# Linear attention in two chained feed-forward stages: the queries' maxima taken by VectorE transposes, and the keys' chain put ahead of them

## What is computed

```python
def phi(x):                                   # per head: 576 x 64 -> 576 x 256
    proj = x @ w_phi                          # 64 x 128
    proj = proj - max(abs(proj), axis=-1)
    return concat([exp(proj), exp(-proj)])
q_p, k_p = phi(q), phi(k)
kv  = einsum('bhsf,bhsd->bhfd', k_p, v)
z   = sum(k_p, axis=tokens)
att = (q_p @ kv) / (q_p @ z + 1e-06)          # heads side by side: 576 x 512
# first feed-forward stage (x_prev is x shifted by one token)
xk = mu_k * x + (1 - mu_k) * x_prev;  xr = mu_r * x + (1 - mu_r) * x_prev
y  = sigmoid(xr @ w_r) * (relu(xk @ w_k) ** 2 @ w_v)
# second stage: 512 -> 1024, a convolution over 3 tokens as a gate, 1024 -> 512
h = relu(y @ w_in);  out = (h * sigmoid(conv3(h))) @ w_out
```

## Time and profile before

| | us |
|---|---|
| median of 3 runs | 1418.75 (1409.08 to 1427.29) |
| the profiled execution | 1417.62 |
| its span | 1415.8 |
| TensorE busy (PE) | 1360.0 (96%) |
| VectorE busy (DVE) | 672.6 (48%) |
| ScalarE busy (ACT) | 626.6 (44%) |
| mean granted TensorE clock | 0.984 |
| first tile matmul of batch 0 starts at | 94.37 |
| second phase starts at about | 990 |

### The profile page before, as it was taken

One profiled execution on the slowest core, in us unless ns is written; L12 is line 12 of the kernel. 1 busy time (PEld: TensorE's weight loads), 2 busy tenths in 40 slices (PEclk: granted clock), 3 DMA queues, 4 the chain that ended last, 5 costly groups with the idle time before them and its releaser, 6 DMA issues. The chain is left out here.

```text
span 1415.8 us, 26326 instructions
## 1 busy us (share of the span) xinstructions
PE 1360.0 (96%) x10368; PEld 1211.6 (86%) x10368; DVE 672.6 (48%) x1047; ACT 626.6 (44%) x1111; POOL 13.5 (1%) x18
## 2 busy tenths in 40 slices
PE   5879999999999999999999999998899999999998
PEld 4668899889888889888988888998788988998997
DVE  5444244334433624442544362451757556655753
ACT  3536345454352534545445353443444443433532
POOL 0000000000000000000000000000300000000000
PEclk9879999999999999999999999999999999999999
DMA  5411202202212120220221212030310210110101
GB/s 165 124 45 40 58 27 77 63 20 69 61 45 70 40 58 26 62 78 19 70 54 53 69 41 58 25 116 22 93 64 1 71 64 30 41 63 30 41 30 38
DMA packets 94579, 78.60 MB, mean 56 GB/s; under 512 B 64656, under 2 KB 72976, under 8 KB 93456
## 3 DMA queue, kind: packets, MB, share of 16 engines
q1 hardware_dynamic: 94480, 77.10, 18.2%
HBM read 57.75 MB, written 19.02 MB: 54 GB/s over the span
## 5 line engine op out<-in xcount | busy, mean ns | idle before, releaser
L472 PE MATMUL psm<-xk_hi,wk_hi 128*128 128x288 f32 x512 | 158.6, 310 | 15.1 <-issue 6.9
L969 PE MATMUL psh<-y_hi,win_hi 128*128 128x288 f32 x512 | 153.9, 301 | 13.4 <-ACT h L1054 9.0
L818 DVE TENSOR_TENSOR k_lo<-square,k_hi 128x288 fp32r<-128x288 f32 x128 | 58.7, 458 | 221.3 <-ACT square L683 221.3
L472 PE MATMUL psm<-k_hi,wv_hi 128*128 128x288 f32 x512 | 154.4, 302 | 0.0
L472 PE MATMUL psm<-xk_lo,wk_hi 128*128 128x288 f32 x512 | 153.7, 300 | 0.0
L472 PE MATMUL psm<-xk_hi,wk_lo 128*128 128x288 f32 x512 | 153.2, 299 | 0.0
L970 PE MATMUL psh<-y_lo,win_hi 128*128 128x288 f32 x512 | 152.2, 297 | 0.0
L971 PE MATMUL psh<-y_hi,win_lo 128*128 128x288 f32 x512 | 151.6, 296 | 0.0
L472 PE MATMUL psm<-k_lo,wv_hi 128*128 128x288 f32 x512 | 151.1, 295 | 0.0
L472 PE MATMUL psm<-k_hi,wv_lo 128*128 128x288 f32 x512 | 150.8, 295 | 0.0
L1112 DVE SCALAR_TENSOR_TENSOR conv<-h,taps,conv 128x576 f32<-128x576 f32 x64 | 55.2, 863 | 141.3 <-ACT conv L1056 141.3
(11 more groups left out here) (116 smaller groups left out, 2810.9 us busy)
## 6 DMA issues: line engine op xcount, KB each, us to landing
v_nat<-in_v SPq DMA_DIRECT2D x32, 320.0 KB, 3.6
qk<-in_q SPq DMA_DIRECT2D x32, 288.0 KB, 2.9
qk<-in_k SPq DMA_DIRECT2D x32, 288.0 KB, 3.2
den<-den_scr SPq DMA_DIRECT2D x64, 144.0 KB, 3.0
y_scr<-y SPq DMA_DIRECT2D x64, 144.0 KB, 1.8
y<-y_scr SPq DMA_DIRECT2D x8, 1152.0 KB, 5.5
out<-rows SPq DMA_DIRECT2D x32, 256.0 KB, 2.0
den_parts<-den_rows SPq DMA_DIRECT2D x128, 2.2 KB, 1.9
```

The source lines that it names most:

```text
L472: return nc.tensor.matmul(o, lhsT, rhs, start=first, stop=last)
L818: nc.vector.tensor_tensor(k2_lo[:, i, :], square[:, i % 2, :], k2_hi[:, i, :].bitcast(F32), ALU.subtract).then_inc(k2_lo_ready, 1)
L969: nc.tensor.matmul(o, wh, xh, start=first, stop=False, skip_group_check=True)
```

## The change

- `QP`, `M`'s five transposes, `P0` and `P1` go. A new TensorE step `E` (`features_and_keys`) makes the queries' features once, with features on partitions (512 + 64 columns for each head), together with the ten key matmuls, which are woven between them. Three waits on `shared_bank` inside it keep writes to one bank apart.
- The keys' chain comes first on VectorE (`shift_keys`): maximum and subtraction of the two tail blocks (256 elements), then of the eight other blocks (1024 elements).
- The queries' maxima: `QT` (`part_maxima`) on VectorE: two 32x32 block transposes of 576 elements a partition out of PSUM, a reduction over 1152 elements, a copy of 64; then `M`: one TensorE transpose of 128x128; then `spread_maxima` on VectorE: a reduction over 128 elements, a cast, a subtraction, and a product over 576 elements that makes `max_blocks`. ScalarE's copy of the maxima goes.
- `KV` stands right behind `M`, ahead of `PICK`, whose input VectorE makes in `spread_maxima`; then `PICK` (`subtract_maxima`): four matmuls over the full height of the array, 512 + 64 + 64 + 512 columns, which add the negative maxima to the features. Then four exponentials, one for each head and sign (2 x 2 of 576 elements as before).
- `DEN` and `NUM` work on chunks of 64 + 512 and 512 + 64 columns in place of 288 + 288. The denominator is copied only when `NUM` is through.
- The list of steps becomes E, QT, EK, M, KV, PICK, DEN, NUM, with tiles behind E, EK, PICK (3200 ns each: two tiles) and NUM (1600: one tile), and 4000 in place of 6000 ns of tiles ahead of the first. Nothing of batch 1 is done in the front any more.

```diff
-FILL_NS = {"QP": 2200, "M": 1600, "P0": 3500, "P1": 2600}
-FIRST_FILL, LAST_FILL, RC_AFTER, DV_AFTER = 6000, 1600, 3500, 9000
+FILL_NS = {"E": 3200, "EK": 3200, "PICK": 3200, "NUM": 1600}
+FIRST_FILL, RC_AFTER, DV_AFTER = 4000, 3800, 9500
...
-        steps += [(s, p) for s in ("KP", "M", "EK", "P0", "KV", "P1", "DEN", "NUM")]
+    return [(s, p) for p in range(PAIRS) for s in ("E", "QT", "EK", "M", "KV", "PICK", "DEN", "NUM")]
...
+        def features_and_keys(p, a):
...
+            key_tile(0, TT - 1).then_inc(shared_bank, 1)
+            feature_chunk(1, 1, True)
+            feature_chunk(0, 0, True)
+            await_(pe, shared_bank, 3 * PAIRS, a, 3 * p + 1)
+            key_tile(1, TT - 1).then_inc(shared_bank, 1)
+            key_tile(0, 0)
+            key_tile(1, 0)
+            await_(pe, shared_bank, 3 * PAIRS, a, 3 * p + 2)
+            feature_chunk(0, 1, True).then_inc(shared_bank, 1)
+            key_tile(1, 1)
+            key_tile(0, 1)
+            await_(pe, shared_bank, 3 * PAIRS, a, 3 * p + 3)
+            feature_chunk(1, 0, False).then_inc(raw_features, 1)
+            for t in range(2, TT - 1):
+                for h in range(2):
+                    last = key_tile(h, t)
+            last.then_inc(k_projected, 1)
...
+        def part_maxima(p, a):
+            for h in range(2):
+                nc.vector.transpose(q_turn[:, h, :], q_cols(h, p, a)).then_inc(q_turned, 1)
+            await_(dve, q_turned, 2 * PAIRS, a, 2 * p + 2)
+            await_(dve, max_turned, PAIRS, a, p)
+            nc.vector.tensor_reduce(q_part[:].rearrange("p (h c) -> p h c", h=4)[:, 0:2, 0:TOK],
+                                    q_turn[:].rearrange("p h (j f) -> p h j f", f=32), AX.X, ALU.max,
+                                    apply_absolute_value=True).then_inc(q_part_once, 1)
+            await_(dve, q_part_once, PAIRS, a, p + 1)
+            nc.vector.tensor_copy(q_part[:, P // 2:P], q_part[:, 0:P // 2]).then_inc(q_part_ready, 1)
+
+        def spread_maxima(p, a):
+            await_(dve, max_turned, PAIRS, a, p + 1)
+            nc.vector.tensor_reduce(q_max[:], turned_max(p, a).rearrange("q (i t) -> q t i", i=4), AX.X, ALU.max).then_inc(q_max_ready, 1)
...
+            await_(dve, features, PAIRS, a, p)
+            nc.vector.tensor_tensor(max_blocks[:], own_block[:].unsqueeze(2).to_broadcast([P, TOK, 32]),
+                                    q_max_split[:].bitcast(F32).unsqueeze(1).to_broadcast([P, TOK, 32]), ALU.mult).then_inc(blocks_ready, 1)
...
+            for h in range(2):
+                for chunk in CHUNKS[h]:
+                    cols = slice(*chunk)
+                    last = mm(q_cols(h, p, a)[:, cols], pick[:, h, :], max_blocks[:].rearrange("q j t -> q (j t)")[:, cols], False, True)
...
         def copy_den(p, a):
-            await_(act, den_summed, PAIRS, a, p + 1)
+            await_(act, attended, PAIRS, a, p + 1)
...
-                if m is None and kind in ("QP", "KP", "P1") and pieces < len(PIECES):
+                if m is None and kind in ("M", "KV", "NUM") and pieces < len(PIECES):
```

More of the change, by code:

```diff
@@ L48, in attention_steps @@
 def attention_steps():
-    steps = [("QP", 0)]
-    for p in range(PAIRS):
-        steps += [(s, p) for s in ("KP", "M", "EK", "P0", "KV", "P1", "DEN", "NUM")]
-        steps += [("QP", p + 1)] if p + 1 < PAIRS else []
-    return steps
+    return [(s, p) for p in range(PAIRS) for s in ("E", "QT", "EK", "M", "KV", "PICK", "DEN", "NUM")]
 def first_attention_steps():
-    steps = [("QP", 0), ("KP", 0)]
+    steps = [("E", 0)]
     for p in range(PAIRS):
         last = p == PAIRS - 1
-        def ahead(s):
-            return [(s, 0, "next") if last else (s, p + 1)]
         def before(s):
             return [(s, p - 1)] if p else []
-        steps += [("M", p)] + before("RC") + [("P0", p), ("EK", p)] + ahead("QP")
-        steps += [("KV", p), ("P1", p)] + before("DV") + ahead("KP") + [("DEN", p), ("NUM", p)]
+        steps += [("EK", p), ("QT", p)] + before("RC") + [("M", p), ("KV", p), ("PICK", p)] + before("DV")
+        steps += [] if last else [("E", p + 1)]
+        steps += [("DEN", p), ("NUM", p)]
         if last:
@@ L340, in batches @@
         work(None, (None, 0), first_attention_steps())
[L341 removed]
+        work((None, 0), (None, 1), iteration(True, True))
         with eng.Fori(1, LAST) as c:
@@ L394, in work @@
         def work(m, a, steps):
-            if a is not None and not second_of(a):
+            if a is not None:
                 load_qk(0, a)
@@ L471, in mm @@
         def mm(o, lhsT, rhs, first, last):
-            return nc.tensor.matmul(o, lhsT, rhs, start=first, stop=last)
+            return nc.tensor.matmul(o, lhsT, rhs, start=first, stop=last, skip_group_check=True)
         def three(o, w_parts, x_parts, first, last):
@@ L479, in three @@
             return mm(o, wl, xh, False, last)
[L481 to L497, removed]
@@ L499, in turn_maxima, with key_tile, feature_chunk @@
-        def turn_maxima(p, a):
[L500 to L513, removed]
-            for h in range(2):
[L515 to L519, removed]
+        def features_and_keys(p, a):
+            await_q_psum(pe, p, a)
+            await_(pe, kvz_copied, PAIRS, a, p)
+            await_(pe, q_loaded[p % 2], 16 * (PAIRS // 2), a, 16 * (p // 2 + 1))
+            await_(pe, k_loaded[p % 2], 16 * (PAIRS // 2), a, 16 * (p // 2 + 1))
+            tails, keys = k_tail(p, a), k_main()
+            def key_tile(h, t):
+                own = slice(D * h, D * h + D)
+                o = tails[:, h, :] if t == TT - 1 else keys[:, h, t, :]
+                return mm(o, qk[own, p % 2, 1, P * t:P * t + P], phi[own, :], True, True)
+            def feature_chunk(h, chunk, first):
+                own, cols = slice(D * h, D * h + D), slice(*CHUNKS[h][chunk])
+                return mm(q_cols(h, p, a)[:, cols], phi[own, :], qk[own, p % 2, 0, cols], first, False)
+            key_tile(0, TT - 1).then_inc(shared_bank, 1)
[15 more added lines that the diff above has]
+            last.then_inc(k_projected, 1)
```

241 lines of the change are left out of this document (117 added, 124 removed).

## The result

The changed kernel took 1473.66 us (median of 4 runs, 1470.80 to 1487.35); the kernel before, on the same chip, 1423.02 (4 runs, 1409.08 to 1428.69). The ratio is 1.039, with a 95% interval of 1.029 to 1.049. The profiled execution took 1474.48 (span 1472.6), 57 more than the 1417.62 of before. I had forecast 1485, with a range of 1395 to 1535, and slower as the likeliest.

What follows compares the result with a forecast made beforehand. It took TensorE's summed stage work to bound the first tile phase, and a chain over all engines the front. 1417.6 - 33.6 (work) + 33.6 (wait) + 56 (clock) + 12 (front) = 1485.6 us, given as 1485, range 1395 to 1535.

Steps and rivals of the forecast that it cites:

- the clock: Among tiles, TensorE's clock falls to 1.2 GHz after two waits before M per iteration, 4.0 us each: +56 us (0 to +110).
- the front: Before the tiles, QT behind a weight piece delays M and KV starts at 1.2 GHz: +12 us (0 to +25).
- TensorE's work: TensorE's stages shrink from 12.44 to 11.27 us a pair, less batch 1's first E: -33.6 us (-11 to -48).
- The wait before M: Among tiles, M waits for VectorE's QT, queued behind `k_lo`: 4.8 us per iteration, seven times, +33.6 us.
- Dense tiles come sooner: Clock price: KV follows as at 76 us but dense tiles come sooner, so 4.0 us a fall (1.7 to 5.1).
- The pair's +4: In the front, a longer chain to M and slow KV, less shrunken stages, add some 4 us a pair.
- less for the last: In the front, the last pair adds less than the others' some +4 us, having no E behind it.
- NUM's copies: A wait of TensorE at E for the numerator's copy, costed at nothing: NUM's one tile covers the copies.
- The keys' load: A wait at E for the DMA, costed at nothing: load issued at the loop's turn, ahead of three K tiles.
- That the clock holds: Rival, among tiles: waits before M come but are too short to lower the clock; 1430 us, chance 0.23.
- That the chain is covered: Rival, VectorE between E and M: QT ends in time, TensorE never stands, clock kept; 1387 us, chance 0.17.

Runs made afterwards that it cites:

- e2: Changed kernel with one tile between E and QT and three between QT and M, instead of two and two: 1407.04 us, ratio 0.992 to the kernel before.
- e3: Changed kernel with one more tile between M and KV at pairs 0 and 3, the longest waits: 1465.76 us, ratio 1.034 to the kernel before.
- e5: Kernel before the change, with the two tiles between P0 and KV moved behind P1, so KV waits: 1558.25 us, ratio 1.100.
- e4: Changed kernel with the front's weight pieces behind QT, M and KV in place of M, KV and NUM: 1469.65 us, median of 4 runs.
- e8: e2 with PICK ahead of KV, one tile between M and PICK and one behind KV: 1573.40 us, ratio 1.109 to the kernel before.
- e9: e2 with PICK right behind M, then KV, and both tiles behind KV: 1683.42 us, ratio 1.187 to the kernel before.
- e6: Changed kernel with the edits of e2 and e4 together: 1395.89 us, ratio 0.984 to the kernel before.
- e1: Changed kernel with the tiles between E and QT put behind QT: 1426.66 us, ratio 1.007 to the kernel before.
- e7: e6 with 5600 ns of tiles in place of 4000 ahead of an iteration's first E: 1412.24 us, ratio 0.996 to the kernel before.

## Why the prediction was right

The sign, the mechanism and, within 0.8%, the time came out, and by the terms named. The largest misses were the clock, 13.5 us too high, and the front, 5.6 too low; they have opposite signs, so part of the closeness is luck.

- **TensorE's work, -33.6.** Measured -35.3. The stages: E 2.77 (180.33 - 177.56; predicted 2.57), M 0.17 (0.15), KV 4.39 (4.50), PICK 0.77 (0.63), DEN and NUM 3.18 (3.42). Sum 11.28 against my 11.27. The 0.25 I had added for halves of unequal size was not there: 3.17 before, 3.18 now. E and PICK, each sized too low, made up for it.
- **The wait before M, +33.6.** Measured 29.1 in 21 waits: 1.61 to 1.70, 0.86, 0, 1.61, where I had 1.7, 1.15, 0.25, 1.7. The unmeasured operation, the block transpose, was placed right by the row of its size:

```profile
L754 DVE STREAM_TRANSPOSE q_turn<-ps 128x576 f32<-128x576 f32 x60 | 42.9, 752 | 0.0
```

- **The clock, +56.** Measured 42.5 for the falls after M (44.0 with the turns of the loop). I had 14 falls of 4.0; there were 8 of 5.3 on average (10.2 us at 1.2 GHz cost 5.1, once 13.6). Two errors half cancel. The count failed: not each wait of 1.7 costs the clock. And the price was too low: it is that of the fall at 76 us in the front, my upper end. "Dense tiles come sooner" did not shorten it; at 375 us KV and PICK at 1.2 GHz took 9.8 us together. The count rested on a reading that left something out: I took the 1.42 us before KV at 75.35 as enough by itself, but TensorE had also waited 0.84 us at 70.43 and 0.79 at 71.93. Whether those helped the clock down is not shown. e2, e3 and e5 show the cause, e4 that the count differs from run to run.
- The Trainium skill ("TensorE: Matmul & The Clock Gate", section "Why this matters for your kernels"), which warns only of long pauses between bursts, would have made this term nothing and the time about 1430. The changed kernel, the pauses of 1.28 in e3, e5 and e8 speak against it for fp32 stages of 65 columns or PICK behind the pause. With a tile behind it, 14 pauses of 1.6 to 1.7 us in e3 agree with it. The pauses of e9, 2.97 to 4.30 us, are long ones, and their falls do not speak against it.
- **The front, +12.** Measured +17.6, first tile at 110.48 for my 105. The pair's +4 was right (24.1 against 20.0), and so was its cause: e4 and e6 take the piece out from ahead of QT, and 15 us come back. The step that failed is "less for the last": its M also waits 6.47 behind a piece, where before it waited 0.84, so the distance from M to M grew there from 17.1 to 24.1.
- **Costed at nothing.** NUM's copies: no wait at E for them. The keys' load: 1.9 us in three turns, and up to 7 in e3. All waits at the turns of the loop together (`y`, `xk_lo`, the load, `relu`) are 10.0 us, against 8.6 before: as good as nothing, as costed.
- **The rivals.** That the clock holds (1430) did not occur: it fell after 8 of the 14 long waits. That the chain is covered (1387) is what e2 came near to by moving one tile, and e6 with the pieces moved too: 1407 and 1396. In the kernel as it was changed it did not occur.

## What to carry to other kernels

When an operation moves to another engine, place it behind what is queued there and not only by its own duration: here one tile's `k_lo` ahead of QT decided over 66 us. Ask of each new pause on TensorE what follows it, and price it with the clock: 1.7 us of waiting mostly cost 5 us more when small fp32 matmuls followed, and nothing more when a dense tile did. A kernel whose pauses sit where the clock may or may not fall also scatters, so read the granted clock and the count of falls before an edit is judged by its time.

## What I had not expected of the hardware

- After equal pauses of 1.6 to 1.7 us before M and KV the clock fell 8 times of 14 in one execution and 12 of 14 in another (e4, unchanged there). In the two together it fell 13 times of 14 after pair 0's pause and 7 of 14 after pair 3's. Shorter pauses: after 1.28 four times of seven (e3), after 0.83 to 1.04 three of seven (e1), after 0.85 never in those two executions but once of seven in e7. Why some pairs lose the clock and others do not stays open.
- A fall with KV behind it lasted 10.2 us at 1.2 GHz or more among the tiles of the changed kernel, and 6.8 to 13.7 in e1, e3, e5 and e7; with dense tiles behind it 3.4, once 6.8 (the turns of the loop in e3 and e7, as the earlier trace rows shows at 451).
- A 512 + 64 split of 576 columns cost TensorE nothing against 288 + 288: 3.18 and 3.17 us for the 32 records of DEN and NUM.
